# Delta rule and two MoE layers: two low weight parts made by TensorE ahead of the first solve, added unread products, and a last store cut in three

## What is computed

```python
def _attn_ref(q, k, v, beta):
    k_n = k / (np.linalg.norm(k, axis=-1, keepdims=True) + 1e-06)
    ...
    for t in range(S):
        kt, vt, bt = (k_n[:, :, t], v[:, :, t], beta[:, :, t, None])
        y[:, :, t] = np.einsum('bhd,bhde->bhe', q[:, :, t], state)
        v_old = np.einsum('bhde,bhd->bhe', state, kt)
        state = state + bt[:, :, :, None] * np.einsum('bhd,bhe->bhde', kt, vt - v_old)

def _moe_ref(x, w_in, w_out):
    h = x @ w_in
    g = np.where(h >= 1, h, np.where(h <= -1, 0.0, (h + 1) ** 2 / 4))
    return g @ w_out

def _moe2_ref(x, w_in, w_out):
    r = np.maximum(x @ w_in, 0.0)
    return (r * r) @ w_out
```

## Time and profile before

| | |
|---|---|
| median of 3 runs | 1013.21 us (1013.2 to 1013.45) |
| the profiled execution's own time | 1011.66 us |
| its span, first to last instruction | 1008.5 us |
| mean granted clock | 0.975 |
| TensorE busy | 966.4 us (96%) |
| VectorE busy | 593.7 us (59%) |
| ScalarE busy | 411.6 us (41%) |
| DMA | 50.91 MB, mean 50 GB/s |

### The profile page before, as it was taken

The page is one execution under the profiler, slowest core; times in us unless marked ns, Lnnn a source line. Parts: engine busy times, 40 slices in busy tenths (PEclk is TensorE's granted clock), DMA queues, the critical chain, the costliest instruction groups (busy, mean ns, idle before and its releaser), DMA issues.

```text
span 1008.5 us, 24126 instructions
## 1 busy us (share of the span) xinstructions
PE 966.4 (96%) x10400; PEld 796.3 (79%) x10400; DVE 593.7 (59%) x1118; ACT 411.6 (41%) x728; POOL 9.5 (1%) x17
## 2 busy tenths in 40 slices
PE   4379999999999999999999999999999999999997
PEld 4268788888888888888888888888888888888886
DVE  6888978786877677768635774433434334333332
ACT  4458544433433344443435554323333233332332
POOL 1000000000000000000000000000000000000000
PEclk7589999999999999999999999999999999999999
DMA  7143133003200320020003511001010010000000
GB/s 234 44 138 106 59 98 101 9 18 85 83 10 19 93 75 11 20 70 32 3 13 107 176 63 63 1 1 63 1 63 1 1 63 1 31 1 1 32 1 31
DMA packets 28376, 50.91 MB, mean 50 GB/s; under 512 B 2288, under 2 KB 15728, under 8 KB 28272
## 3 DMA queue, kind: packets, MB, share of 16 engines
q1 hardware_dynamic: 28272, 49.39, 15.3%
HBM read 39.94 MB, written 9.44 MB: 49 GB/s over the span
## 4 chain that ended last, share of the span: by engine, by line
PE 92%; DVE 5%; issue 1%; ACT 1%; DMA 0%; ACTq 0%; DVEq 0%
PE psum L966 39%; PE psum L942 38%; PE psum L795 2%; PE psum L838 2%; PE psum L773 2%; PE psum L818 2%; PE psum L809 2%; DVE tmp L1066 1%; DVE x_inv L1069 1%; PE psum L894 1%; PE psum L866 1%; PE psum L871 1%; PE psum L879 1%; PE psum L751 1%; PE psum L734 1%
## 5 line engine op out<-in xcount | busy, mean ns | idle before, releaser
L966 PE MATMUL psum<-g_hi,w 128*128 128x512 f32 x1152 | 392.1, 395 | 0.0
L942 PE MATMUL psum<-x_hi,w 128*128 128x512 f32 x1152 | 386.6, 390 | 1.2 <-DVE x_lo L1166 1.2
L1184 DVE TENSOR_TENSOR g_lo<-act_g,g_hi 128x512 fp32r<-128x512 f32 x192 | 132.6, 691 | 210.7 <-ACT g_hi L650 210.7
L966 PEld LDWEIGHTS psum<-g_hi,w 128*128 128x128 f32 x1152 | 216.2, 188 | 50.7 <-issue 2.0
L942 PEld LDWEIGHTS psum<-x_hi,w 128*128 128x128 f32 x1152 | 216.2, 188 | 46.8 <-issue 1.4
L650 ACT ACTIVATE g_hi<-act_g 128x512 fp32r<-128x512 f32 x192 | 121.4, 632 | 273.4 <-PE psum L966 238.8
L966 PE MATMUL psum<-g_lo,w 128*128 128x512 f32 x576 | 224.6, 390 | 0.0
L942 PE MATMUL psum<-x_lo,w 128*128 128x512 f32 x576 | 224.1, 389 | 0.0
L1178 DVE TENSOR_TENSOR act_g<-act_g 128x512 f32<-128x512 f32 x96 | 66.4, 692 | 112.9 <-ACT act_g L643 112.9
L942 PEld LDWEIGHTS psum<-x_lo,w 128*128 128x128 f32 x576 | 108.1, 188 | 22.1
L966 PEld LDWEIGHTS psum<-g_lo,w 128*128 128x128 f32 x576 | 108.2, 188 | 20.6
(11 more groups left out here) (83 smaller groups left out, 568.9 us busy)
## 6 DMA issues: line engine op xcount, KB each, us to landing
kt_sb<-in_k_t SPq DMA_DIRECT2D x24, 256.0 KB, 4.2
qt_sb<-in_q_t SPq DMA_DIRECT2D x24, 256.0 KB, 3.6
kn_sb<-in_k_n SPq DMA_DIRECT2D x20, 256.0 KB, 4.0
ring<-in_v_s SPq DMA_DIRECT2D x24, 192.0 KB, 2.8
between_layers<-y_out SPq DMA_DIRECT2D x6, 768.0 KB, 4.0
x_sb<-between_layers SPq DMA_DIRECT2D x6, 768.0 KB, 5.6
result<-y_out SPq DMA_DIRECT2D x6, 768.0 KB, 3.9
wi_st<-in_w_in SPq DMA_DIRECT2D x7, 384.0 KB, 3.9
```

Source lines behind the costliest of these rows:

```text
L942: ins = pe.matmul(h_ps[n % 2][:, :], w_in_part(layer, f // GW, part)[:, kt, fs], x[:, kt, :], start=(kt == 0 and j == 0), stop=(kt == KT - ...
L966: ins = pe.matmul(acc[kt][:, :], w_out_part(layer, f // GW, part)[:, f % GW, ds], g[n % 2][:, :], start=(f == 0 and j == 0), stop=(f == NF ...
L1184: dve.tensor_tensor(g_lo[n % 2][:, :], act_g[n % 2][:, :], g_hi[n % 2][:, :].bitcast(F32), ALU.subtract).then_inc(g_lo_ready, 1)
```

## The change

1. Two squares, `eye` (the identity) and `minus_eye` (minus it), are made on POOL ahead of the memset of `u_sb`.
2. The low parts of groups 0 and 1 are no longer made by VectorE but by TensorE: `low_parts` adds eye by the staged weights and minus_eye by their high part in PSUM, all f32, 384 columns at a time in banks 4 and 6 in turn; ScalarE copies each half out (`low_out`). They stand on TensorE behind the diagonal blocks of chunk 1.
3. `keep_busy` multiplies eye by the mask and writes a PSUM bank that nobody reads from it: one product at the start of each of the last eight inverse steps, two behind the last, one behind each substitute, and one ahead of the first step.
4. The four `keys_by_queries` stand behind the four solves, one behind each; `masked` moves along on VectorE.
5. Of solve(0), ScalarE copies three batches out and VectorE one.
6. SyncE's loads are put in another order: groups 0 and 1 ahead of the values and queries, groups 3 and 2 ahead of the query load that waits for the first `keys_by_queries`.
7. The last second product counts each of its three accumulators by itself; ScalarE copies each as it is done, and each is stored by itself (256 KB instead of 768 KB once).

```diff
+        eye = sa("eye", [P, P])
+        minus_eye = sa("minus_eye", [P, P])
         gd = sa("gd", [P, NH, BLK])
...
+        def flat_part(g, part, out_part, half_of):
+
+            return weights[0][g][:, part, out_part, half_of * GW * DM // 2:(half_of + 1) * GW * DM // 2]
+
         def w_out_part(layer, g, part):
...
         h_ps = bank[0:2]
+        low_ps = bank[4], bank[6]
         acc_ps = [bank[2:5], bank[5:8]]
...
+        eye_ready = sem("eye_ready")
+        low_done = sem("low_done")
+        low_half = sem("low_half")
+        tail_done = sem("tail_done")
         mask_ready = sem("mask_ready")
...
                 load_kt(m)
+            load_weights(0, 0, w_in1, w_out1)
+            load_weights(0, 1, w_in1, w_out1)
+            for k in range(1, RING):
+                load_v(k)
             for m in range(QUERIES):
                 load_qt(m)
-            load_weights(0, 0, w_in1, w_out1)
-            for k in range(1, RING):
-                load_v(k)
-            load_weights(0, 1, w_in1, w_out1)
+            load_weights(0, EARLY, w_in1, w_out1)
             for m in range(2):
                 load_kn(m)
+            load_weights(0, 2, w_in1, w_out1)
             load_qt(B - 1)
-            load_weights(0, EARLY, w_in1, w_out1)
-            load_weights(0, 2, w_in1, w_out1)
             for k in range(NB):
...
                     load_between(t + 2)
-                store_out(t)
-            sp.wait_ge(out_stored, 32 * NTT)
+                if t < NTT - 1:
+                    store_out(t)
+            for kt in range(KT):
+                sp.wait_ge(acc_ready, KT * (2 * NTT - 1) + kt + 1)
+                sp.dma_start(out.rearrange("(k p) (t j) -> t p k j", p=P, j=TT)[NTT - 1][:, kt, :], y_out[:, kt, :]
+                             ).then_inc(out_stored, 16)
+            sp.wait_ge(out_stored, 16 * (2 * NTT - 1 + KT))
...
                                base=0, pattern=[[1, P]], channel_multiplier=-1).then_inc(mask_ready, 1)
+            for square, value in ((eye, 1.0), (minus_eye, -1.0)):
+                pool.memset(square[:, :], value).then_inc(eye_ready, 1)
+            pool.wait_ge(eye_ready, 2)
+            for square in (eye, minus_eye):
+                pool.affine_select(out=square[:, :], in_=square[:, :], compare_op=ALU.is_equal, fill=0.0,
+                                   base=0, pattern=[[1, P]], channel_multiplier=-1).then_inc(eye_ready, 1)
             pool.memset(u_sb[:, :, :], 0.0).then_inc(u_zero, 1)
...
                     act.activation(x_set(layer, t)[0][:, kt, :], x_from(layer, t, kt), ACT.Copy).then_inc(x_hi_ready, 1)
+
+            def low_out(g, out_part):
+
+                for half_of in range(2):
+                    act.wait_ge(low_done, 4 * g + 2 * out_part + half_of + 1)
+                    act.activation(flat_part(g, LOW, out_part, half_of), low_ps[half_of][:, 0:GW * DM // 2], ACT.Copy
+                                   ).then_inc(w_lo_ready if half_of else low_half, 1)
...
             def drain(layer, t):
-                act.wait_ge(mm2_done, first_of(layer, t + 1))
+                act.wait_ge(mm2_done, min(first_of(layer, t + 1), 2 * STEPS - 1))
                 wait(act, out_stored, 16 * (layer * NTT + t))
...
                 for kt in range(KT):
+                    if layer and t == NTT - 1:
+                        act.wait_ge(tail_done, kt + 1)
                     act.activation(y_out[:, kt, :], acc_of(layer, t)[kt][:, :], ACT.Copy).then_inc(acc_ready, 1)
...
                 gram_out(m)
-            for hp in range(2):
-                gd_out(1, hp)
+            split_weights(0, 0, 0)
+            split_weights(0, 0, 1)
+            gd_out(1, 0)
+            split_weights(0, 1, 0)
+            split_weights(0, 1, 1)
+            gd_out(1, 1)
+            low_out(0, 0)
+            low_out(0, 1)
+            scaled_first(0)
+            low_out(1, 0)
+            low_out(1, 1)
+            for k in range(1, NB):
+                scaled_first(k)
             for k in range(NB):
-                scaled_first(k)
-            for g in range(2):
-                split_weights(0, g, 0)
-                split_weights(0, g, 1)
-            for k in range(NB):
-                solved(k, 0)
-                solved(k, 1)
+                for b in range(3 if k == 0 else 2):
+                    solved(k, b)
                 if k == 0:
...
                 else:
-                    pe.wait_ge(scaled0, H)
-                    pe.wait_ge(gd_ready, 2)
+                    pe.wait_ge(w_lo_ready, 4)
                 if n == 0:
...
                 if c == 0:
-                    pe.wait_ge(gd_ready, 2)
+                    pe.wait_ge(low_half, 4)
                 elif b < 2 and c + 1 < NC:
...
                 ins.then_inc(y_done, 1)
+
+            def low_parts(g, out_part):
+
+                at, turn = stage_of(0, g)
+                pe.wait_ge(eye_ready, 4)
+                pe.wait_ge(ws_loaded[at], 32 * turn)
+                pe.wait_ge(w_hi_ready, 2 * g + out_part + 1)
+                pe.wait_ge(gd_ready, 2)
+                for half_of in range(2):
+                    wait(pe, w_lo_ready if half_of else low_half, 2 * g + out_part)
+                    out_ps = low_ps[half_of][:, 0:GW * DM // 2]
+                    whole_part = staged(0, g)[out_part].rearrange("p a c -> p (a c)")
+                    pe.matmul(out_ps, eye[:, :], whole_part[:, half_of * GW * DM // 2:(half_of + 1) * GW * DM // 2],
+                              start=True, stop=False)
+                    pe.matmul(out_ps, minus_eye[:, :], flat_part(g, HIGH, out_part, half_of).bitcast(F32),
+                              start=False, stop=True).then_inc(low_done, 1)
+
+            def keep_busy(columns, out_ps):
+
+                if out_ps is bank[4]:
+                    pe.wait_ge(low_half, 4)
+                pe.matmul(out_ps[:, 0:columns], eye[:, :], later[:, :].unsqueeze(1).to_broadcast([P, columns // P, P]),
+                          start=True, stop=True)
...
                                         start=(f == 0 and j == 0), stop=(f == NF - 1 and j == 2))
-                ins.then_inc(mm2_done, 1)
+                    if n == 2 * STEPS - 1:
+                        ins.then_inc(tail_done, 1)
+                if n < 2 * STEPS - 1:
+                    ins.then_inc(mm2_done, 1)
...
                 diagonals_of(1, hp)
-            for m in range(B - 1):
-                keys_by_queries(m)
+            for g in range(2):
+                low_parts(g, 0)
+                low_parts(g, 1)
+            pe.wait_ge(mask_ready, 2)
+            for j in range(23, BLK - 1):
+                pe.wait_ge(inv_chain, 2 * j + 2)
+                keep_busy((3 if j < 27 else 2) * P, bank[4])
+            pe.wait_ge(inv_chain, CH)
+            keep_busy(4 * P, bank[4])
+            keep_busy(3 * P, bank[4])
             for k in range(NB):
                 solve(k)
-                if k == 2:
-                    keys_by_queries(B - 1)
+                keys_by_queries(k)
                 if k < NB - 1:
                     substitute(k + 1)
+                    keep_busy(2 * P, bank[4])
             for m in range(B):
...
             gram_of(B)
+            keep_busy(4 * P, bank[1])
...
                 if k == 2:
-                    split_weights(0, 0, 0)
-                if k == 3:
                     masked(1)
-                solved_first(k, 2)
+                if k:
+                    solved_first(k, 2)
                 solved_first(k, 3)
...
                 if k == 2:
-                    split_weights(0, 0, 1)
+                    masked(2)
                 if k < NB - 1:
                     residual(k + 1)
-            masked(2)
-            split_weights(0, 1, 0)
-            split_weights(0, 1, 1)
             masked(B - 1)
```

## The result

The changed kernel takes 1010.08 us, the median of 8 executions (1009.0 to 1011.2), against 1013.21 before; the ratio is 0.9972 with a 95% interval of 0.9961 to 0.9982. That is 2.8 to 3.1 us gained where 5.1 were forecast, in the stated range, and clear of noise. Its profiled execution took 1011.17 us with a span of 1009.4. One execution of one experiment (early_old_loads), its profiled one, took 4,965 us, with its 512-column products at some 1.5 us each; it is left out, and so that kernel has no trace to compare.

The account below looks back on a forecast made before the run. TensorE was taken as full from 68.4 to 1003 us, leaving only the stretches before and after. 4.0 us ahead, less 0.4 for lateness, plus 1.5 tail gave 5.1 us: 1013.21 to 1008.1 us, range 1006.3 to 1010.8.

Parts of the forecast that it names:

- head: Stretch ahead of the first MoE product: 4.0 us gained by a warm TensorE and lighter VectorE, less 0.4 for late low parts.
- tail: After the last product: 0.97 us gained on copies and 0.5 on a smaller last store, 1.5 in all.
- the fourth rival: Waits bind elsewhere, the head brings nothing and the tail its 1.5 us: 1011.7 us; chance 0.03.
- signs of being wrong: low_parts ending after 38 us, a solve taking 1.5 us, or TensorE waiting in the first steps for group 2 or 3.
- The price of a product by eye: In low_parts, two passes a record: 384 columns take 0.67 us warm and 1.29 cold.
- The clock in low_parts: TensorE's clock rises after 5.0 us of unbroken work in low_parts, which then ends at 36.8 us.
- The slower rival: The clock never rises in low_parts and the substitution starts 13 us late: about 1025 us; chance 0.07.
- The late low parts: Rival: late clock or longer code stall delays solve(0) by 2 to 3.5 us: 1010.1 to 1011.6 us; chance 0.18.
- The hand-overs of the substitution: From solve(0) at 42.85 us, warm steps with VectorE setting residual(1) and residual(2); first product at 64.45 us.
- keys_by_queries(k), 16 records, and the 256-column products lie in gaps: In the substitution, keys take 0.9 us of 1.5 to 1.7 us gaps, the 256 columns 0.46 of 0.8.
- the second rival: The clock falls again in the substitution, making solves, substitutes and outputs cold: 1009.5 to 1011 us; chance 0.07.

Follow-up runs that it names:

- early_old_loads: one_group with keys_by_queries(0) to (2) before the inverse's end, 512 unread columns in their old places, group 3's load ahead of group 2's again; ratio 0.9921.
- early_two_copies: one_group with keys_by_queries(0) to (2) before the inverse's end, 512 unread columns in their places, solve(0) copied two batches each by ScalarE and VectorE; 0.9919, 1004.42 us.
- group3_later: Changed kernel with weight group 3's load moved behind group 2's; ratio 0.9959 to the kernel before, 1008.51 us.
- early_two_groups: Changed kernel with keys_by_queries(0) to (2) behind low_parts replacing the eight unread products of the inverse steps, 512 unread columns in their old places; 0.9913, 1003.68 us.
- early_idle: one_group with keys_by_queries(0) to (2) before the inverse's end and no unread columns behind solves 0, 1 and 3; ratio 0.9961, 1008.72 us.
- one_group: group3_later with only group 0's low parts on TensorE, group 1's on VectorE, and unread products from the inverse's 19th step; ratio 0.9960, 1009.21 us.
- gaps_filled: group3_later with 384 more unread columns behind each keys_by_queries of the substitution; ratio 0.9969, 1010.36 us.

## Why the prediction was right, and where it was not

The time lay in the range and the direction was right, but by another sum than the one on record: 3.6 us of head and 1.5 of tail were forecast, 0 and 2.4 measured. That is in part luck. With nothing from the head and the 1.5 us of tail the time is 1011.7, above the range of 1006.3 to 1010.8; it is the figure of the fourth rival (0.03), which put it down to waits that bind elsewhere and not to the clock. The tail's 0.9 us more brought the time back into the range. Two of the three signs of being wrong came, too: low_parts ended at 38.0, right at the bound named, and two solves took 1.50 us.

- **The price of a product by eye** was right. A product of 384 columns, a pair of records, starts 0.64 us behind the one before it warm (forecast 0.67) and 1.28 cold (1.29), so each of the two records is two passes over 384 columns at 2.4 or 1.2 GHz.
- **The clock in low_parts** rose 3.7 us after its start at 25.3, sooner than the 5.0 us taken. Over the ten traces of kernels with low_parts in which the granted clock shows the rise it took 2.9 (early_two_copies) to 5.8 us (group3_later), so the 5.0 was one value of a spread. The slower rival, a clock that never rises there, is out in every trace.
- **The late low parts** were under-rated. The stall grew by 1.66 us as described, low_parts ended at 38.0 instead of 36.8, and 6.0 us behind it, as worked out, came solve(0): 1.07 us late, not 0.4. But early_two_groups shows that this lateness need not be: it has the longest stall, and still its solve(0) comes 0.14 us behind xc, since its keys_by_queries replace the eight unread products.
- **The hand-overs of the substitution** were right, once TensorE is warm. early_two_groups has solve(1) 4.87 us behind solve(0), where the forecast's starts are 4.65 apart; substitute(2) 7.22 (7.0), solve(3) 13.16 (13.15), the first output 15.44 (15.4), the first product 21.2 (21.6). All along VectorE or ScalarE sets the pace, as was said of residual(1) and residual(2).
- **The step that failed** is "keys_by_queries(k), 16 records, and the 256-column products lie in gaps", at 56 ns a record, and with it the 0.07 given to a clock that falls again. The 0.9 us hold only while the clock does; in the changed kernel it fell at the second of them. Then each keys_by_queries takes 2.08 us in front of a substitute or an output, and the stall in keys_by_queries(1) adds 0.9. This is the second rival, under-priced: from solve(0) to the first product the trace shows 27.4 us where 21.6 were forecast, 5.8 more, and the rival's 1009.5 to 1011 lie 1.4 to 2.9 above the forecast. I counted one solve and one substitute cold (1.2 us) and some cold outputs, and not that the keys stand in the way, nor that the clock stays down until the outputs, 17 us later.
- **What made it fall** is shown in part. The unread products in the gaps behind the solves hold the clock as a rule: with them and the keys out of the way, four kernels are at 0.9913 to 0.9921, and the mean granted clock of each of their 18 executions is 0.991 to 0.993 (the start of the kernel included); early_idle, which lacks only them, is at 0.9961 with 0.983 to 0.986 in its six executions, and the changed kernel has 0.983 to 0.990 in eight. It is no certainty: in early_two_copies the clock fell for 3.4 us all the same. The keys in the same gaps don't hold it (one_group), keys and 384 columns together only at times (gaps_filled), and moving the keys away by itself doesn't (early_idle). No run here tells whether it is the 128 rows instead of 48, or one long product instead of eight short ones, that counts.
- **The stall is not what made it fall in the changed kernel**: the clock fell at 49.5 us and TensorE stood from 50.9 on. In seven of the nine traces of kernels with low_parts in which it falls in the substitution, no stall of this kind comes ahead of it; only in gaps_filled and in group3_later (at 57.5 us) does it fall behind one. It stays open that "issue" is fetching of code; for it speak the same place in the program in different traces, and the lengthening by loads.
- **The tail** was mis-sized, not misread: about the 0.97 us for the copies as forecast, and 1.4 for the store (3.5 us to 2.1) where 0.5 were taken. The landing times of loads were the wrong neighbour for a store. By the Trainium skill (DMA: Bandwidth & Descriptors, Anatomy of one DMA) it was 1.2 us, an estimate, nearer than the rows came, though the 2.6 us that the same formula makes of a 256 KB transfer are more than the 2.1 measured; the page fitted it to transfers issued from GpSimd, and these stores are SyncE's.

## What to carry to other kernels

Useful work that is put into the gaps of a latency-bound chain must be short at the slow clock too, for it may meet it: here it paid to put the real work ahead of the chain, where nobody waits, and into the gaps wide products that nobody reads (6 us from the changed kernel to early_two_groups). Look at every copy and store behind the last product: cutting these in pieces by accumulator brought 2.4 us, and all the rest of the change nothing. Where a change has two ends, time each alone; here the sum hid it.

## What the runs showed of the hardware that was not expected

- Work that the profile shows as unbroken need not raise the clock. In the changed kernel TensorE is busy 12.79 of 12.80 us from 51.8 on, with solves, substitutes and keys for the most part, and the clock is 0.50 until the outputs are under way, while low_parts, products over 128 rows and 128 columns of the array, raised it in 3.7 us (2.9 to 5.8 over ten traces):

```profile
25.30:29.10 3.80, 3.80 (x6) 2.14 (x7) 3.53 (x9) 0.49 (x1) 0.00 (x0) 0.51 0.01 2
...
51.80:64.60 12.80, 12.79 (x296) 10.35 (x296) 6.17 (x11) 2.70 (x6) 0.00 (x0) 0.50 0.14 35
```

- The clock can fall without a long idle stretch: in the changed kernel TensorE was busy 4.37 of the 5.48 us from solve(0) to 49.40, its longest wait 0.60 us, and the clock fell right behind.
- Stores of 256 KB landed in 2.1 us, those of 768 KB in 3.5 to 4.3.
